# Seven products in the first MLP: two of three superblocks of a fused attention and MLP kernel

## The chip, the cores and the metric

The kernel runs on one core of a Trainium2 chip. The metric is device time in microseconds (us) of one execution; a smaller number is better.

## What is computed

Attention comes first: for 4 batches, 8 heads, 576 positions and 64 channels, the sum of a softmax attention over positions averaged in fours and of a local one with a band of 7 positions. Its output, as 2304 tokens of 512 channels, goes through two MLPs, all in float32:

```python
x = attn_out.transpose(0, 2, 1, 3).reshape(B * S, H * D)     # 2304 x 512
a = x @ w1;  b = x @ w2                                      # 512 -> 1024
y = ((a * b) @ w3) @ w_out                                   # 1024 -> 1024 -> 512
h = maximum(maximum(y @ u1, y @ u2), y @ u3)                 # 512 -> 768
out = h @ u_out                                              # 768 -> 512
```

## The kernel before, in words

Everything is kept transposed, channels on the 128 partitions and tokens along the free axis; `xy` holds the 2304 tokens of x, then of y, in four planes. Every float32 product is made of three TensorE matmuls on halves: an operand is split into a rounded high part (ScalarE, a copy into fp32r, L1033) and the rest (GpSimd, sometimes VectorE: a subtraction, L1187 or L784), and `split_product` (L596 to L598) adds high by high, high by low and low by high in PSUM. One operand is the stationary weight tile of 128 by 128, the other streams.

The work runs in three stages.

- **Prologue.** w3 @ w_out is formed once, as `w3o` (`product`), in 64 pieces of three matmuls, while the attention of the first batch (units 0 to 3, a unit is two heads of one batch) runs between the pieces.
- **First MLP**, five blocks of tokens, four of 512 and one of 256 (`T0`, `TN`). Of each block, L1 makes a and b (`first_mlp`, kind "L1": 8 tiles f of 128 hidden channels, twice for w1 and w2, 4 tiles k of the inner dimension, three matmuls each: 192), ScalarE copies a into `gate` (`gate_copy`), VectorE multiplies it by b (L856, `gate_product`), ScalarE and GpSimd split the product into `h_t`; L2 (96 matmuls) multiplies by `w3o` and ScalarE writes y over x. The attention units 4 to 15 are interleaved. A "part" is six matmuls of this stage.
- **Second MLP**, three superblocks of 768 tokens (`SUPER`, `HALF` = 384). Here each 2x2 block product of tiles is done with seven products instead of eight (`pair_products`): numbers e = 1 to 7, each of one summed weight tile and one summed operand. Products are added in PSUM and by VectorE. The summed and split weights are made once, in 24 steps n (`PREPS`), during the first MLP: SP loads 128 by 512 raw numbers (`load_raw`, L536), ScalarE copies them to PSUM (`copy_raw`), VectorE makes the four sums (L863 to L868, `combine`), ScalarE rounds (`high_wb`), VectorE subtracts (L784, `low_wb`), and SP stores 128 by 1792 numbers to DRAM in three DMAs (L545, `store_ready`). They are read back from there through a ring in `weights_split` (`load_group`, L558) in every superblock. The buffers of the steps lie in the memory of the attention, so `load_raw(0)` waits for the last unit (`x_ready`).

The order of the instructions on each engine is written out ahead of time: every job has a position, in parts of the stage, and each engine runs its own jobs sorted by position (`in_order`), waiting on semaphores. `position` gives it for the attention, `parts_of_mlp`, `after_parts` and `x_splits` for the MLP and `preparations` for the steps n. SP issues all DMAs, in its order too; a DMA whose wait isn't over holds up all DMAs behind it.

## Time and profile before

| | |
|---|---|
| median of 3 runs | 692.66 us (692.54 to 693.13) |
| the profiled execution | 692.93 us, span 691.1 us |
| TensorE busy | 684.6 us, 99% of the span |
| weight loads, beside the matmuls | 609.5 us |
| VectorE, ScalarE, GpSimd busy | 378.9, 244.0, 263.5 us |
| DMA | 131.73 MB, mean 191 GB/s |

The 1.8 us between the span and the device time lie ahead of the first and behind the last instruction. A matmul row's own duration holds its way through the array and overlaps the next one's; what a matmul costs TensorE is the distance between two starts.

### The profile page before, as it was taken

The numbers are of one execution on the slowest core, as the hardware profiler recorded it, in microseconds if no ns is written. First come the engines' busy times: TensorE is split into PE (matmuls) and PEld (weight loads), VectorE is DVE, ScalarE is ACT, GpSimd is POOL, SyncE is SP. The second block draws the span as 40 slices with busy tenths as digits, with TensorE's granted clock in tenths as the row PEclk, the third lists the DMA queues.
The fourth block names the chain that finished last, engine by engine and source line by source line (L and its number), as shares of the span: only waits on it lengthen the run. The fifth ranks groups of instructions, "written<-read, shape, count | busy, mean of one in ns | idle before, by whom it ended". The sixth has DMA issues, their size and how long they took to land.

```text
span 691.1 us, 15782 instructions
## 1 busy us (share of the span) xinstructions
PE 684.6 (99%) x6656; PEld 609.5 (88%) x6656; DVE 378.9 (55%) x707; ACT 244.0 (35%) x514; POOL 263.5 (38%) x240
## 2 busy tenths in 40 slices
PE   9999999999999999999999999999999999999998
PEld 7787788888888888888888999999999999999997
DVE  4464555433544354435666326676576767756673
ACT  5565333323333233245665334122431223412231
POOL 6989422410415112240222137123570335904341
PEclk9999999999999999999999999999999999999999
DMA  9884122222212222049999666777399765897732
GB/s 314 272 281 137 55 78 78 63 93 60 79 44 77 78 69 65 24 135 324 340 325 319 239 226 243 248 233 263 121 360 354 229 251 162 319 372 252 233 119 92
DMA packets 43798, 131.73 MB, mean 191 GB/s; under 512 B 4944, under 2 KB 8272, under 8 KB 42960
## 3 DMA queue, kind: packets, MB, share of 16 engines
q1 hardware_dynamic: 43728, 130.73, 55.4%
q8 instruction: 52, 0.85, 0.5%
q14 instruction: 18, 0.15, 0.1%
HBM read 103.97 MB, written 26.74 MB: 189 GB/s over the span
## 4 chain that ended last, share of the span: by engine, by line
PE 95%; POOL 3%; DMA 1%; DVE 0%; issue 0%; SPq 0%; ACT 0%; DVEq 0%
PE psum L596 29%; PE psum L597 28%; PE psum L598 28%; PE psum L635 3%; PE psum L613 2%; PE psum L606 2%; POOL second_split L1187 2%; PE psum L644 1%; PE psum L623 1%; DMA xy<-wa 1%; POOL product_split L1187 1%; POOL weights_split L1187 1%; DVE sums L939 0%; POOL attention L1191 0%; SPq L513 0%
## 5 line engine op out<-in xcount | busy, mean ns | idle before, releaser
L596 PE MATMUL psum<-second_split,weights_split 128*128 128x384 f32 x402 | 135.1, 336 | 2.3 <-issue 0.9
L598 PE MATMUL psum<-second_split,weights_split 128*128 128x384 f32 x402 | 134.3, 334 | 0.0
L597 PE MATMUL psum<-second_split,weights_split 128*128 128x384 f32 x402 | 134.3, 334 | 0.0
L1187 POOL TENSOR_TENSOR h_split<-gate,h_split 128x512 fp32r<-128x512 f32 (+1 forms) x40 | 47.1, 1178 | 223.6 <-ACT h_split L1033 223.6
L1187 POOL TENSOR_TENSOR second_split<-xy,second_split 128x384 fp32r<-128x384 f32 x75 | 82.0, 1118 | 129.1 <-ACT second_split L1033 129.1
L596 PE MATMUL psum<-x_split,weights_split 128*128 128x512 f32 (+1 forms) x320 | 120.8, 377 | 0.0
L597 PE MATMUL psum<-x_split,weights_split 128*128 128x512 f32 (+1 forms) x320 | 117.9, 369 | 0.0
L598 PE MATMUL psum<-x_split,weights_split 128*128 128x512 f32 (+1 forms) x320 | 117.9, 368 | 0.0
L596 PEld LDWEIGHTS psum<-second_split,weights_split 128*128 128x128 f32 x402 | 75.5, 188 | 4.5 <-issue 1.8
L597 PEld LDWEIGHTS psum<-second_split,weights_split 128*128 128x128 f32 x402 | 75.5, 188 | 0.0
L598 PEld LDWEIGHTS psum<-second_split,weights_split 128*128 128x128 f32 x402 | 75.5, 188 | 0.0
L596 PEld LDWEIGHTS psum<-x_split,weights_split 128*128 128x128 f32 x320 | 60.3, 189 | 11.8 <-issue 1.8
L598 PEld LDWEIGHTS psum<-x_split,weights_split 128*128 128x128 f32 x320 | 60.4, 189 | 10.3
L597 PEld LDWEIGHTS psum<-x_split,weights_split 128*128 128x128 f32 x320 | 60.4, 189 | 9.2
L856 DVE TENSOR_TENSOR gate<-gate,psum 128x512 f32<-128x512 f32 (+1 forms) x40 | 25.2, 631 | 69.4 <-PE psum L598 69.4
L1033 ACT ACTIVATE attention<-psum 128x896 fp32r<-128x896 f32 (+2 forms) x56 | 39.5, 706 | 61.7 <-PE psum L644 26.9
L596 PE MATMUL psum<-h_split,product_split 128*128 128x512 f32 (+1 forms) x160 | 59.8, 374 | 0.0
L597 PE MATMUL psum<-h_split,product_split 128*128 128x512 f32 (+1 forms) x160 | 58.9, 368 | 0.0
L598 PE MATMUL psum<-h_split,product_split 128*128 128x512 f32 (+1 forms) x160 | 58.9, 368 | 0.0
L1033 ACT ACTIVATE sums<-psum 128x384 f32<-128x384 f32 x33 | 16.2, 491 | 101.4 <-PE psum L598 101.3
L1033 ACT ACTIVATE second_split<-xy 128x384 fp32r<-128x384 f32 x75 | 37.7, 523 | 39.4 <-DVE xy L946 12.6
L1033 ACT ACTIVATE h_split<-gate 128x512 fp32r<-128x512 f32 (+1 forms) x40 | 23.5, 589 | 77.7 <-DVE gate L856 77.6
(111 smaller groups left out, 1157.1 us busy)
## 6 DMA issues: line engine op xcount, KB each, us to landing
weights_split<-weights_stream SPq DMA_DIRECT2D x39, 768.0 KB, 4.8
weights_split<-weights_stream SPq DMA_DIRECT2D x54, 512.0 KB, 4.8
weights_stream<-attention SPq DMA_DIRECT2D x48, 256.0 KB, 2.9
xy<-wa SPq DMA_DIRECT2D x40, 256.0 KB, 4.7
attention<-qk SPq DMA_DIRECT2D x16, 576.0 KB, 4.1
weights_stream<-attention SPq DMA_DIRECT2D x24, 384.0 KB, 3.2
weights_split<-weights_stream SPq DMA_DIRECT2D x6, 1152.0 KB, 5.1
attention<-v_win SPq DMA_DIRECT2D x16, 384.0 KB, 3.5
```

The lines of the kernel that those rows point to most:

```text
L596: pe.matmul(out, lhs[:, 0], rhs[:, 0], start=first, stop=False, skip_group_check=read_between)
L597: pe.matmul(out, lhs[:, 0], rhs[:, 1], start=False, stop=False, skip_group_check=read_between)
L598: return pe.matmul(out, lhs[:, 1], rhs[:, 0], start=False, stop=last, skip_group_check=read_between)
L606: mm = pe.matmul(score_d[rows, j, :], qkd[rows, 0, DSTEP * j:DSTEP * j + DROWS], qkd[rows, 1, :], start=True, stop=True)
L613: mm = pe.matmul(score_l[TW * i:TW * (i + 1), h, g, :], qk_sb[rows, 0, Q0[t]:Q0[t] + TW], qk_sb[rows, 1, K0[t]:K0[t] + TW], start=True, st ...
L623: mm = pe.transpose(turned_d[:, kt, P * j:P * (j + 1)], prob_d[:, j, TD * kt:TD * (kt + 1)], ident)
L635: mm = pe.matmul(bank(4 + i)[D * h:D * (h + 1), PV + TQ * g:PV + TQ * (g + 1)], v_sb[rows, g, D * h:D * (h + 1)], prob_t[rows, h, g, own:o ...
L644: mm = pe.matmul(pv_down[D * h:D * (h + 1), :], vd[:, kt, D * h:D * (h + 1)], own, start=kt == 0, stop=kt == 1)
L856: dve.tensor_tensor(at, at, bank(2 * (f % 2) + 1)[:, 0:TN[n]], ALU.mult).then_inc(h_ready, 1)
L1033: return act.activation(out, src, ACT.Copy)
L1187: return pool.tensor_tensor(out, full, high.bitcast(F32), ALU.subtract)
```

## The change

The first MLP's L1 uses seven products too, for tokens 768 to 2303 (superblocks 2 and 3). Tokens 0 to 767 stay plain, in two blocks of 384 (`SUPER`, `HALF`, `T0`, `TN`, `NB`). In these lines PROLOGUE is 64, PARTS 48, so `G_BEGIN` is 160 and `B_BEGIN` 336; for each of the two gated superblocks there are 56 parts of products (`GUNITS` = 8 units, 4 pairs of hidden tiles by w1 and w2, of 7 products of six matmuls), then 32 of L2.

```diff
-T0 = [0, 512, 1024, 1536, 2048]
-TN = [512, 512, 512, 512, 256]
-NB, TMAX = len(T0), 512
+SUPER, HALF = 3, 384
+T0 = [0, HALF]
+TN = [HALF, HALF]
+NB, TMAX = len(T0), HALF
...
+GP = F1 // 2
+GUNITS = 2 * GP
+GPREPS = GUNITS * KP
+GATED = SUPER - 1
+PRODUCT_W = 2 * KP * P
+PLACES = 9
+GMADE = 3
...
+G_ORDER = ((0, 1), (0, 2), (1, 4), (0, 6), (1, 3), (0, 5), (0, 7))
...
+G_BEGIN = PROLOGUE + PARTS * NB
+G_FIRST, G_PARTS = 7 * GUNITS, 7 * GUNITS + 8 * JO
+B_BEGIN = G_BEGIN + G_PARTS * GATED
...
-VISITS = {"S": 0, "T": 5, "V": 8}
+VISITS = {"S": 0, "T": 5, "V": 8.1}
+
+UNIT_AT = [None] * PAIRS + [PROLOGUE + 1.5 + 9.8 * i for i in range(2 * PAIRS)] + [
+    G_BEGIN - 5 + 15 * i for i in range(PAIRS)]
...
+def gate_preparations(late):
+
+    return [PROLOGUE + 5 + 4.9 * n + late for n in range(GPREPS)]
...
-    return [PROLOGUE + PARTS * 2 + 33.5 + 2.6 * n + late for n in range(PREPS)]
+    return [G_BEGIN + 54 + 3.35 * n + late for n in range(PREPS)]
...
+def gated_loads():
+
+    return [(G_BEGIN - 7 if i < PLACES else G_AT[PRODUCTS[i - PLACES]] + 1.15, ("PRODUCT", i)) for i in range(len(PRODUCTS))]
...
+            def load_gate_raw(n):
+                if n >= GMADE:
+                    sp.wait_ge(gmade_out[(n - GMADE) % 2], GMADE_INC * ((n - GMADE) // 2 + 1))
+                sp.dma_start(gmade_b[n % GMADE].rearrange("p (e two) c -> p e two c", two=2)[:, :, 1, :],
+                             wc[n].rearrange("p (e c) -> p e c", e=4)).then_inc(wc_in[n % GMADE], 16)
+
+            def store_gate(n):
+                to = products_dram(n // KP, n % KP)
+                sp.wait_ge(wc_hi, n + 1)
+                for r in range(2):
+                    some = slice(4 * r, min(4 * r + 4, 7))
+                    sp.dma_start(to[:, 0, some, :], ghigh_b[n % 2][:, r, 0:some.stop - some.start, :].bitcast(F32)).then_inc(
+                        gmade_out[n % 2], 16)
+                sp.wait_ge(wc_lo, n + 1)
+                sp.dma_start(to[:, 1], gmade_b[n % GMADE][:, 0:7, :]).then_inc(gmade_out[n % 2], 16)
+
+            def load_product(i):
...
+                if i >= PLACES:
+                    sp.wait_ge(product_done, i - PLACES + 1)
...
+                sp.dma_start(places[i % PLACES].bitcast(F32), product_dram(7 * (q % GUNITS) + IN_PIECE.index(e))).then_inc(
+                    place_in[i % PLACES], 16)
...
+            for step in in_order(loads(), gated_loads(),
+                                 [(max(at, PROLOGUE + 1), ("GATE_RAW", n)) for n, at in enumerate(gate_preparations(-4.5))],
+                                 [(at, ("GATE_OUT", n)) for n, at in enumerate(gate_preparations(5.5))],
+                                 [(at, ("RAW", n)) for n, at in enumerate(preparations(-4.5))],
+                                 [(at, ("READY", n)) for n, at in enumerate(preparations(4))]):
+                run[step[0]](*step[1:])
...
+            def gate_product(q, e):
...
+                pe.wait_ge(place_in[i % PLACES], 16 * (i // PLACES + 1))
...
+                for kp in range(KP):
+                    if u == 0:
+                        pe.wait_ge(xs_lo, 7 * KP * s + X_SPLIT[(e, kp)] + 1)
+                    mm = split_product(out, lhs[:, kp], xs_r[(e, kp)], kp == 0 and e in (1, 2, 5), kp == KP - 1, True)
+                mm.then_inc(product_done, 1)
...
+            def gate_result(q, tile):
...
+                if tile == (1, 0):
...
+                    dve.tensor_tensor(to, to, a, ALU.mult).then_inc(g_summed[tile], 1)
+                    return
...
+                if q % 2 == 0:
+                    wait_for_results(dve, q)
+                    dve.tensor_tensor(to, kept, from_bank, ALU.add).then_inc(g_summed[tile], 1)
+                else:
+                    dve.tensor_tensor(kept, kept, from_bank, ALU.add).then_inc(g_summed[tile], 1)
+                    dve.wait_ge(g_summed[tile], q + 1)
+                    dve.tensor_tensor(to, to, kept, ALU.mult).then_inc(gated_by[tile], 1)
...
+            def combine_wc(n):
+
+                made = gmade_b[n % GMADE]
+                pool.wait_ge(wc_in[n % GMADE], 16 * (n // GMADE + 1))
+                pool.tensor_tensor(made[:, 2, :], made[:, 7, :], made[:, 5, :], ALU.add)
...
+            def low_wc(n):
+                made = gmade_b[n % GMADE].rearrange("p (r e) c -> p r e c", r=2)
+                pool.wait_ge(wc_hi, n + 1)
+                low(made.bitcast(F32R), made, ghigh_b[n % 2]).then_inc(wc_lo, 1)
```

Beside what is shown: the sums of w1 and w2 for the seven products are made in 16 steps (`GPREPS`) during the two plain blocks. Each loads 128 by 512 numbers, GpSimd makes four sums and, after ScalarE has rounded (`high_wc`), the low parts; three DMAs store 128 by 1792 numbers to `gate_weights_stream` in DRAM. `load_product` reads 128 by 512 numbers for each of the 112 products into one of nine places, and product i + 9 can only be loaded when product i is done. Every product is loaded anew for superblock 3. The seven operands of x are made for each gated superblock (`split_xs`, `make_x`: 14 copies, 14 subtractions, 8 differences). ScalarE copies products 1, 6 and 7 (and every second 4) out of PSUM (`keep`), and VectorE adds and multiplies (`gate_result`). The gated h goes to `gated_r`, and L2 takes it in eight groups of 384 tokens (`last_layer`).

SP, in the products of superblock 3. L545 and L768 are `store_ready` before and now, L536 and L759 `load_raw`, L752 is `load_product`. Before:

```order
L545 DMA weights_stream<-attention 128x512 [waits wb_lo]
L545 DMA weights_stream<-attention 128x768
L545 DMA weights_stream<-attention 128x512
L536 DMA attention<-wb 128x512 [waits s_made]
L545 DMA weights_stream<-attention 128x512 [waits wb_lo]
```

and now:

```order
L768 DMA weights_stream<-attention 128x512
L752 DMA weights_split<-gate_weights_stream 128x512 [waits product_done]
L759 DMA attention<-wb 128x512 [waits s_made]
L752 DMA weights_split<-gate_weights_stream 128x512 [waits product_done] x2
L768 DMA weights_stream<-attention 128x512 [waits wb_lo]
L768 DMA weights_stream<-attention 128x768
L768 DMA weights_stream<-attention 128x512
L752 DMA weights_split<-gate_weights_stream 128x512 [waits product_done]
```

The loads of products now stand between the stores of the steps n. From the first load of superblock 3's second nine to the end of the steps there are 47 product loads, 14 steps' stores and 12 raw loads.

VectorE, in the same place. L1094 is `low_wb`, L1177 to L1182 are `combine`, L1238, L1248 and L1250 `gate_result`. Before (L784 is `low_wb`, L863 to L868 `combine`):

```order
L784 TENSOR_TENSOR attention<-psum,attention 128x7x128 [waits wb_hi]
L863 TENSOR_TENSOR psum<-psum,attention 128x128 [waits raw_copied]
L864 TENSOR_TENSOR psum<-psum,attention 128x128
L866 TENSOR_TENSOR psum<-psum,attention 128x128 [waits s1_made]
L868 TENSOR_TENSOR psum<-attention,psum 128x128 [waits s2_made]
```

and now:

```order
L1094 TENSOR_TENSOR attention<-psum,attention 128x7x128 [waits wb_hi]
L1238 TENSOR_TENSOR xy<-xy,psum 128x384 [waits g21_kept,product_done]
L1177 TENSOR_TENSOR psum<-psum,attention 128x128 [waits raw_copied]
L1178 TENSOR_TENSOR psum<-psum,attention 128x128
L1180 TENSOR_TENSOR psum<-psum,attention 128x128 [waits s1_made]
L1182 TENSOR_TENSOR psum<-attention,psum 128x128 [waits s2_made]
L1248 TENSOR_TENSOR gate<-gate,psum 128x384 [waits product_done,kept16]
L1250 TENSOR_TENSOR xy<-xy,gate 128x384 [waits g12_summed]
```

The results of the products, for which TensorE waits, now stand behind `low_wb`, which waits for ScalarE.

## Rows read from the trace of the kernel before

**Rows 1.** The page: busy time and, in 40 slices, the granted clock.

```profile
PE 684.6 (99%) x6656; PEld 609.5 (88%) x6656; DVE 378.9 (55%) x707; ACT 244.0 (35%) x514; POOL 263.5 (38%) x240
...
PEclk9999999999999999999999999999999999999999
```

**Rows 2.** Who TensorE waited for: total us, times, longest.

```profile
PE psum L720 <- DVE gate L900: 1.1, 1, 1.1
PE psum L596 <- issue: 0.9, 1, 0.9
PE psum L596 <- POOL second_split L1187: 0.8, 2, 0.4
PE psum L596 <- DVE sums L939: 0.6, 3, 0.2
```

**Rows 3.** Timeline, TensorE, 512 columns, from 295.76: start us, us.

```profile
295.76 0.39 PE L598 MATMUL psum<-x_split,weights_split 128*128 128x512 f32 x1
...
301.88 0.39 PE L598 MATMUL psum<-h_split,product_split 128*128 128x512 f32 x1
```

**Rows 4.** The same in the second MLP, 384 columns.

```profile
429.73 0.33 PE L596 MATMUL psum<-second_split,weights_split 128*128 128x384 f32 x1
...
433.89 0.33 PE L596 MATMUL psum<-second_split,weights_split 128*128 128x384 f32 x1
```

**Rows 5.** The same in the block of 256 tokens.

```profile
397.42 0.28 PE L598 MATMUL psum<-x_split,weights_split 128*128 128x256 f32 x1
...
408.58 0.28 PE L598 MATMUL psum<-x_split,weights_split 128*128 128x256 f32 x1
```

**Rows 6.** The chain that ended last: start us, us, what.

```profile
50.39 1.08 PE psum L635 x71
51.47 0.64 PE psum L644 x8
...
53.71 0.88 PE psum L606 x12
54.59 0.95 PE psum L613 x63
...
59.89 0.66 PE psum L623 x6
...
412.10 12.28 POOL second_split L1187 x10
```

**Rows 7.** Windows: us, busy of each engine, clock, DMA share, GB/s.

```profile
core 0: us, PE busy (x) PEld busy (x) DVE busy (x) ACT busy (x) POOL busy (x), PEclk, DMA share, GB/s
3.00:17.00 14.00, 13.90 (x167) 11.65 (x166) 7.52 (x15) 7.96 (x18) 10.31 (x9) 1.00 1.04 363
69.00:295.00 226.00, 225.98 (x3364) 182.30 (x3363) 104.39 (x205) 71.34 (x174) 65.40 (x58) 1.00 0.22 66
...
320.00:370.00 50.00, 50.00 (x222) 41.42 (x221) 33.17 (x78) 28.52 (x46) 10.67 (x9) 1.00 0.95 332
514.00:529.00 15.00, 14.11 (x81) 13.82 (x81) 7.01 (x14) 1.36 (x3) 1.96 (x3) 1.00 1.03 407
```

**Rows 8.** Groups by shape, VectorE: busy us, mean ns, idle before.

```profile
L946 DVE TENSOR_TENSOR xy<-xy,sums 128x384 f32<-128x384 f32 x54 | 36.2, 671 | 1.9
L784 DVE TENSOR_TENSOR attention<-psum,attention 128x896 fp32r<-128x896 f32 x24 | 26.2, 1092 | 26.3 <-ACT attention L1033 26.3
...
L976 DVE TENSOR_TENSOR sums<-sums,psum 128x384 f32<-128x384 f32 x18 | 9.9, 552 | 7.9 <-PE psum L598 7.9
...
L868 DVE TENSOR_TENSOR psum<-attention,psum 128x128 f32<-128x128 f32 x24 | 7.1, 296 | 0.8
```

**Rows 9.** The same, GpSimd.

```profile
L1187 POOL TENSOR_TENSOR h_split<-gate,h_split 128x512 fp32r<-128x512 f32 x32 | 41.2, 1288 | 192.4 <-ACT h_split L1033 192.4
...
L1187 POOL TENSOR_TENSOR h_split<-gate,h_split 128x256 fp32r<-128x256 f32 x8 | 5.9, 737 | 31.3 <-ACT h_split L1033 31.3
```

**Rows 10.** Who SP's DMA queue waited for: total us, times, longest.

```profile
SPq L545 <- DVE attention L784: 36.2, 24, 2.3
```

372 lines of the change are left out of this document (337 added, 35 removed), and 2 rows, old and new, of the table FOLLOWS.

## The prediction

> **What bounds the kernel now.** I read the page first: TensorE is busy 99% of the span and its granted clock stands at full speed in every slice [rows 1]. Then who TensorE waited for: 0.9 us, 0.8 us in two waits, 0.6 us in three, and the start [rows 2]. So no transfer and no other engine sets the time. It is the sum of TensorE's matmuls, and a change is worth what it takes from that sum, less the waits that it makes.
>
> What a matmul costs is read from starts in the timeline. 512 columns: (301.88 - 295.76) / 27 = 0.2267 us [rows 3]. 384 columns: (433.89 - 429.73) / 24 = 0.1733 us [rows 4]. 256 columns: (408.58 - 397.42) / 93 = 0.1200 us [rows 5]. The three lie on one line: 0.4167 ns a column and 13.3 ns for each matmul. Narrower matmuls thus cost something by themselves.
>
> **TensorE's sum.** Removed are the five blocks of the first MLP: 4 x 288 matmuls of 0.2267 us and 288 of 0.12 us, 261.1 + 34.6 = 295.7 us. In their place stand two plain blocks, 2 x 288 x 0.1733 = 99.8 us, and two gated superblocks of 336 + 192 matmuls, 2 x 528 x 0.1733 = 183.0 us, in all 282.9 us. The difference is **-12.8 us**. (The product saves 36,864 columns, 15.4 us; 192 more matmuls give 2.6 us back.) Attention, prologue and second MLP keep their matmuls.
>
> The wait of 0.8 us on GpSimd's splits ahead of the second MLP [rows 2, 6] should go: there a chain of ten splits, 12.28 us, followed the last block's h. Now y of superblock 1 is ready from the plain blocks, and most of the 14 splits have positions beside the L2 of superblock 3, 32 parts of 1.04 us. **-0.6 us** on the path; between 0 and -0.8.
>
> **The DMA in superblock 3** is the term that decides. A product uses its weights for one part, 6 x 0.1733 = 1.04 us, and loads 128 x 512 numbers, 0.262 MB. Alone that is 252 GB/s. In superblock 2 the loads of the attention come on top; units stand 15 parts apart, in time 15 x 1.04 + 4.2 = 19.8 us with their own five groups of matmuls (1.08, 0.64, 0.88, 0.95 and 0.66 us, [rows 6]), and move 1.31 MB each (128 x 1152, 128 x 768 and 80 x 1024 numbers): 66 GB/s more. 320 GB/s should pass.
>
> The 24 steps that make the second MLP's weights (0.262 MB read, 0.917 MB stored each) start only after the attention. Before, they ran beside plain blocks: [rows 7] show 332 GB/s and 0.95 of the DMA engines at 320 to 370 us, that is one step per 3.55 us. Now the first ten fall beside the L2 of superblock 2, where TensorE loads nothing, and the other fourteen between the products of superblock 3. SP's order ties them together: a product's load stands behind the stores whose position is earlier.
>
> Follow superblock 3 from position 89, where its first product is done and the tenth can be loaded, to position 141, where product 53 starts: 52 parts, 54.1 us of TensorE. Ahead of product 53 the queue must have moved 45 product loads (11.8 MB), the stores of 13 steps (11.9 MB) and 12 raw loads (3.1 MB): **26.9 MB**, 497 GB/s. No window of the trace has that. What it has: 363 GB/s with rows of about 2 KB a partition and a full queue at 3 to 17 us, 407 GB/s with ring groups of 4 to 6 KB at 514 to 529 us, both with a share of over 1.0 [rows 7]. The steps' window gives 332 / 0.95 = 349 GB/s at full share, and the loads at the start 363 / 1.04 = 349 as well. The new product loads have 2 KB a partition, the stores 2 and 3 KB, so the start's window is nearest, and I take 363 GB/s: 26.9 / 0.363 = 74.1 us, a wait of **+20.0 us**. Bounds: 407 GB/s gives 66.1 us and +12.0; 332 GB/s, the steps' own rate, gives 81.0 us and +26.9. Nine places hold 9.4 us of work, but they are full at position 88 and so are within these numbers; the products go back to one per 1.04 us only when the steps are out.
>
> This term rests on two rates that TensorE never met before, since the ring groups are long and read far ahead. The Trainium skill ("HBM Reference", Specifications (TRN2)) says that a core streaming alone gets about 425 GB/s. The trace has 407 over 15 us for loads alone and less for every stretch with stores; by the page's figure the wait would be an estimated 9 us and the whole about 690.5 us.
>
> **What else the change adds.** VectorE, in the same 52 parts: 13 steps of 1.09 + 4 x 0.296 = 2.27 us, 29.6 us; and for each 14 parts (a pair of units) seven operations on PSUM at 0.55 us and three in SBUF at 0.67 us, 5.9 us, so 21.8 us [rows 8]. 51.4 us of 54.1: it would just fit, and under 74 us of DMA it is covered. If the DMA cover were gone, VectorE would be at 95% and late wherever it waits for ScalarE; that is a part of the rest term below.
>
> GpSimd, in the plain blocks: 256 columns take 0.737 us and 512 take 1.288 [rows 9], so 2.15 ns a column and 0.19 us. A step of the w1, w2 sums has four operations of 128 columns (0.46 us each) and one of 1024 (2.39): 4.2 us. With h, x and the attention's sums about 6.5 us in a step's 4.9 parts, which last 5.1 us and 2.1 us of attention. 0.9 of its time, mostly off the path: h's last tile stands ahead of the next long operation in its order.
>
> The DMA there: 16 steps of 1.18 MB and 8 units of 1.31 MB, 29.4 MB in 78.4 parts and 8 units, 115 us: 256 GB/s. But the stores write pieces of 512 bytes, which no row shows. From below: no wait at 332 GB/s. From above: attention alone shows 66 / 0.22 = 300 GB/s at full share [rows 7], 98 us, still no wait. From the two saturated windows I estimate some 20 ns a row beside the bytes, hence 215 GB/s for such stores and 110 us in all. It stays inside, narrowly.
>
> The attention's chain: in the prologue the turned scores follow 4.35 us behind the scores (55.54 to 59.89) with no wait [rows 2, 6]. Now five parts, 5.2 us, lie between. In two places only one part lies between a unit's values and the next scores; some 0.5 us each.
>
> For these together, **+2 us**, between 0 and 6.
>
> **Sum.** 692.9 (the profiled execution) - 12.8 - 0.6 + 20.0 + 2.0 = 701.5 us. The profiled execution lies 0.3 us over the median of the runs, so I say 701 us: slower. 0.2%, 1.4 us, is about what a measurement of this kernel can tell from no change.
>
> **The rivals.**
> 1. *The queue runs at its ring rate.* Then the wait is 9 to 12 us and the others are small: 692.9 - 13.4 + 12 + 1 = 692.5, down to 690 by the page's rate. For: 407 GB/s was held for 15 us. Against: those were reads of long rows. 17%.
> 2. *Stores and loads hardly hinder each other*, and the sign turns: reads are 14.9 MB and writes 11.9 MB; if only the greater counted, 14.9 / 0.363 = 41 us, under TensorE's 54.1. No wait there, 692.9 - 13.4 + 2 = 681.5. It decides once stores and loads together pass 497 GB/s. For: no window has both directions saturated. Against: the steps' window has 0.95 of the engines busy at 332 GB/s, three quarters of it stores. 12%.
> 3. *The queue is also left empty.* SP waits for `low_wb` before a step's stores, 36.2 us in 24 steps, 1.5 us each [rows 10], and the product loads behind are held up with it; `low_wb` on VectorE and the `gate_result` behind it wait for ScalarE, which waits for older stores. If the queue runs dry half that time, 14 x 0.75 = 10.5 us more: 712; all of it: 722. The small stores of the first steps, if slower than estimated, would end there too. 16%.
> 4. The forecast, 696 to 709: 55%.
>
> **Range and chances.** Rival 2 (12%) and the upper half of rival 3 (8%) are left out: 690 to 714 us. Faster by over 0.2%: rival 2 and a third of rival 1, 18%. Within 0.2%: 8%. Slower: 74%.
>
> **What would show it.** Right: TensorE waits summing to some 20 us between 88 and 146 parts of the stage, released by DMA into `weights_split` from `gate_weights_stream`, in short waits ahead of products, while the DMA share is near 1.0 and the rate 350 to 410 GB/s; TensorE's matmul counts as above and none longer; hardly a wait in superblock 2. Wrong: TensorE waits small there with a rate near 500 GB/s (rival 2); waits released by VectorE or ScalarE with a DMA share under 0.9 (rival 3); a granted clock under 1.0 where TensorE waits, which would make each product longer by an amount that no row here prices.

## The result, and the profile after

The changed kernel takes **719.46 us** (median of 4 runs, 716.67 to 720.53), the kernel before on the same chip 692.89 us (692.54 to 693.20). The ratio is 1.0377, 95% interval 1.0347 to 1.0407: slower, by 26.6 us, where 701 us was forecast. The profiled execution took 716.67 us, its span is 714.9 us (691.1 before).

The page of the changed kernel. Where TensorE was busy for 99% it is now for 96%, its granted clock is no longer full everywhere [rows 1], and the queue moves 180 MB in place of 132:

```profile
PE 686.9 (96%) x6848; PEld 654.2 (92%) x6848; DVE 416.4 (58%) x779; ACT 275.2 (38%) x590; POOL 342.8 (48%) x344
...
PEclk9999999999999999998998899999999999999999
...
GB/s 309 270 280 127 139 248 258 195 247 210 207 242 208 257 262 219 274 299 315 371 406 408 347 217 195 183 258 229 229 227 404 245 221 228 243 404 251 211 144 88
```

Windows over the three parts of the program (columns as in [rows 7]). The first product of superblock 3 starts at 328.79, the second MLP at 447.50. The fourth window begins with the stretch for which the prediction worked out its bytes and ends at 408.0, where the queue runs empty; product 53, the end of that stretch, starts at 411.1:

```profile
0.00:328.79 328.79, 319.75 (x4808) 292.77 (x4809) 188.24 (x369) 156.88 (x355) 215.96 (x223) 0.99 0.77 238
328.79:447.50 118.71, 103.35 (x529) 99.65 (x529) 57.29 (x123) 50.30 (x95) 30.53 (x30) 0.91 0.85 321
447.50:714.90 267.40, 263.75 (x1513) 261.76 (x1512) 170.85 (x289) 68.05 (x140) 96.28 (x91) 1.00 0.68 238
329.80:408.00 78.20, 62.84 (x299) 59.14 (x298) 46.62 (x105) 38.23 (x69) 12.12 (x12) 0.88 1.03 386
```

What each part should take is known. Before, the second MLP began at 424.42; less the 12.8 us of the prediction's first term it should begin at 411.6, and superblock 3, 528 matmuls of 0.1733 us, 91.5 us, should begin at 320.1. So the 23.8 us that the span grew, and the 12.8 us that were saved and lost again, 36.6 us, lie here:

| part | should take | takes | more | TensorE idle |
|---|---|---|---|---|
| up to superblock 3 | 320.1 | 328.8 | 8.7 | 9.0 |
| superblock 3 | 91.5 | 118.7 | 27.2 | 15.4 |
| second MLP | 266.7 | 267.4 | 0.7 | 3.7 |

Idle is the window less TensorE's busy time; in the first and last row a part of it stood there before as well (6.5 us in all). In superblock 3 it leaves 11.8 us that TensorE spent in slower matmuls. Of the 9.0 us idle in the first row, 8.1 lie ahead of 220 us, in the prologue and the plain blocks; the first product of superblock 2 starts at 218.87.

Who TensorE waited for, in place of [rows 2]:

```profile
PE psum L861 <- ACT attention L1392: 6.4, 4, 3.0
PE psum L822 <- issue: 4.8, 3, 4.0
PE psum L822 <- DVE results L1238: 3.0, 1, 3.0
PE psum L822 <- DVE xy L1238: 2.6, 1, 2.6
PE psum L822 <- ACT gate L1392: 2.3, 2, 2.0
PE psum L822 <- ACT parts L1392: 1.8, 4, 0.9
```

No row names a DMA. In superblock 3 TensorE waits for `gate_result` (L1238) and for ScalarE's copies of products (`parts`, `gate`), that is for the banks of PSUM into which the next products go. The first row is the attention's values (L861), in the plain blocks.

The longest wait, 3.98 us, is one of the three under `issue`, for which the profile names no releaser. TensorE's timeline there, at the first wait of superblock 3 (start, us, what, in brackets the idle time ahead):

```profile
330.53 0.33 PE L823 MATMUL psum<-weights_split 128*128 128x384 f32 x1
330.70 0.34 PE L824 MATMUL psum<-weights_split 128*128 128x384 f32 x1
335.02 0.66 PE L822 MATMUL psum<-weights_split 128*128 128x384 f32 x1 [3.98 <-issue]
335.48 0.52 PE L823 MATMUL psum<-weights_split 128*128 128x384 f32 x1
335.80 0.52 PE L824 MATMUL psum<-weights_split 128*128 128x384 f32 x1
```

Two losses stand here. One is the wait. ScalarE's timeline shows what it was for: `high_wb`, waiting for an older store, stood ahead of the copy of a product into `parts`, which ended at 334.91, 0.1 us ahead of TensorE's start:

```profile
333.62 0.92 ACT L1392 ACTIVATE attention<-psum 128x896 fp32r<-128x896 f32 x1 [2.04 <-DMA weights_stream<-attention]
334.43 0.48 ACT L1392 ACTIVATE parts<-psum 128x384 f32<-128x384 f32 x1
```

The other is in the starts behind the wait: 0.32 us apart, where 0.17 us is the full rate. The granted clock of 330 to 340 us was 0.70, a mixture of the full clock and the lower level of 1.2 GHz. Such starts stand in five stretches: behind the waits that ended at 335.02, 358.21 and 378.39 (3.98, 3.05 and 2.59 us), and from 391.85 and 405.31 on, behind shorter waits (1.97 us until 390.73, 1.58 and 0.24 until 405.31). Together they took 9.0 us more than at the full rate. Four windows of 10 us:

```profile
330.00:340.00 10.00, 6.02 (x22) 5.73 (x22) 5.53 (x12) 4.67 (x8) 0.00 (x0) 0.70 0.96 318
350.00:360.00 10.00, 5.77 (x27) 4.90 (x26) 6.88 (x16) 5.08 (x9) 2.03 (x2) 0.89 1.04 394
...
370.00:380.00 10.00, 7.04 (x35) 6.35 (x34) 6.66 (x16) 5.04 (x9) 1.84 (x2) 0.91 1.05 407
390.00:400.00 10.00, 9.24 (x43) 8.98 (x44) 7.46 (x19) 5.87 (x11) 2.48 (x3) 0.83 1.05 404
```

The busy time of TensorE hides this loss, since a slow matmul is busy too: it is in the 118.7 - 91.5 - 15.4 = 11.8 us. These windows also show the DMA engines fully busy at 404 to 407 GB/s with reads and stores mixed.

The chain that ended last, 348 to 379 us (start, us, what). It goes round in the steps that make the second MLP's weights: the stores land, ScalarE rounds the step after next (`high_wb`), VectorE subtracts (`low_wb`, L1094), SP stores (L768). `ready_b` has two buffers, so one round carries two steps:

```profile
348.42 7.06 DMA weights_stream<-attention
355.56 0.93 ACT attention L1392
356.51 1.10 DVE attention L1094
...
358.67 6.73 DMA weights_stream<-attention
...
368.55 7.11 DMA weights_stream<-attention
...
378.64 7.31 DMA weights_stream<-attention
```

A round takes (378.64 - 348.42) / 3 = 10.1 us. The order plans two steps in 2 x 3.35 parts of 1.04 us, 7.0 us. If all seven rounds for the fourteen steps that lie here took as long as these three, they come to 7 x 3.1 = 21.7 us, an estimate: most of the 27.2. The products' copies and sums stand in the same orders as the steps, so TensorE is slowed to the steps' pace.

In the plain blocks another chain ends last. GpSimd works without a gap, ScalarE waits for it with the rounding of the w1, w2 sums, and the unit's `attention` copy, for which TensorE waits 2.96 us, stands behind:

```profile
188.19 2.35 POOL room L1615
190.54 0.97 POOL weights_split L1615
...
192.96 0.46 POOL room L1659
...
193.44 0.03 ACT xy L1392
...
194.91 0.70 ACT attention L1392
...
195.75 1.14 PE psum L861 x69
```

ScalarE's own waits say the same for the whole run:

```profile
ACT attention L1392 <- DMA weights_stream<-attention: 26.9, 14, 3.1
ACT xy L1392 <- POOL room L1659: 26.7, 12, 5.1
```

### The profile page after: what moved, and what is told of

Read it like the earlier page. It is cut to its first block, busy times and chain, and to the rows that moved or that the text cites. A ratio compares the mean times of both kernels' runs of the same rounds, so it can differ in the third digit from the quotient of the medians.

```text
span 714.9 us, 16905 instructions
## 1 busy us (share of the span) xinstructions
PE 686.9 (96%) x6848; PEld 654.2 (92%) x6848; DVE 416.4 (58%) x779; ACT 275.2 (38%) x590; POOL 342.8 (48%) x344
## 4 chain that ended last, share of the span: by engine, by line
PE 82%; DMA 6%; POOL 4%; DVE 2%; issue 2%; ACT 2%; SPq 1%; ACTq 0%; DVEq 0%; POOLq 0%
PE psum L822 25%; PE psum L824 24%; PE psum L823 24%; DMA weights_stream<-attention 5%; PE psum L861 2%; PE psum L839 2%; PE psum L832 2%; PE psum L870 1%; POOL room L1615 1%; PE psum L849 1%; ACT attention L1392 1%; DMA attention<-ident 1%; POOL h_split L1615 1%; DVE attention L1094 1%; SPq L768 1%
## 5 line engine op out<-in xcount | busy, mean ns | idle before, releaser
L1615 POOL TENSOR_TENSOR second_split<-xy,second_split 128x384 fp32r<-128x384 f32 x99 | 103.1, 1058 | 224.8 <-ACT second_split L1392 224.8
L822 PE MATMUL psum<-weights_split 128*128 128x384 f32 x278 | 99.1, 357 | 16.2 <-issue 4.8
L823 PE MATMUL psum<-weights_split 128*128 128x384 f32 x278 | 96.8, 348 | 0.0
L824 PE MATMUL psum<-weights_split 128*128 128x384 f32 x278 | 96.5, 347 | 0.0
L1615 POOL TENSOR_TENSOR weights_split<-xy,weights_split 128x384 fp32r<-128x384 f32 (+1 forms) x65 | 76.3, 1190 | 21.4 <-ACT weights_split L1392 21.3
L822 PEld LDWEIGHTS psum<-weights_split 128*128 128x128 f32 x278 | 55.2, 198 | 21.8 <-issue 21.4
L1392 ACT ACTIVATE second_split<-xy 128x384 fp32r<-128x384 f32 x99 | 49.4, 521 | 41.5 <-DVE xy L1305 12.6
L823 PEld LDWEIGHTS psum<-weights_split 128*128 128x128 f32 x278 | 55.0, 198 | 0.0
L824 PEld LDWEIGHTS psum<-weights_split 128*128 128x128 f32 x278 | 55.0, 198 | 0.0
L822 PE MATMUL psum<-x_split,weights_split 128*128 128x384 f32 x128 | 45.4, 354 | 0.0
L1094 DVE TENSOR_TENSOR attention<-psum,attention 128x896 fp32r<-128x896 f32 x24 | 26.2, 1090 | 30.2 <-ACT attention L1392 30.2
L824 PE MATMUL psum<-x_split,weights_split 128*128 128x384 f32 x128 | 43.3, 339 | 0.0
L823 PE MATMUL psum<-x_split,weights_split 128*128 128x384 f32 x128 | 43.3, 338 | 0.0
L1392 ACT ACTIVATE xy<-psum 128x384 f32<-128x384 f32 x45 | 22.0, 489 | 55.1 <-PE psum L824 51.2
```

What stands on the lines that cost most here:

```text
L822: pe.matmul(out, lhs[:, 0], rhs[:, 0], start=first, stop=False, skip_group_check=read_between)
L823: pe.matmul(out, lhs[:, 0], rhs[:, 1], start=False, stop=False, skip_group_check=read_between)
L824: return pe.matmul(out, lhs[:, 1], rhs[:, 0], start=False, stop=last, skip_group_check=read_between)
L1094: return dve.tensor_tensor(out, full, high.bitcast(F32), ALU.subtract)
L1392: return act.activation(out, src, ACT.Copy)
L1615: return pool.tensor_tensor(out, full, high.bitcast(F32), ALU.subtract)
```

## The experiments

Each kernel is the changed one with the edit shown. Beside the median I give the length of superblock 3 (from its first product to the second MLP) in the profiled execution, since it is freer of what happens elsewhere: where the plain blocks are the same, superblock 3 began at 328.8, 329.7, 332.2, 330.3, 333.7, 332.9 and 332.5 us, a scatter of 5 us that the medians contain. TensorE was idle for 8.8 to 10.3 us up to there in all seven, so the rest of the scatter is in slower matmuls. The profiled execution of the change is the fastest of its four. The kernel before took 692.5 to 693.0 us each time.

| kernel | median us (runs, range) | ratio, 95% interval | superblock 3: us | of it idle | slower matmuls |
|---|---|---|---|---|---|
| the change | 719.46 (4, 716.67 to 720.53) | 1.0377 (1.0347 to 1.0407) | 118.7 | 15.4 | 11.8 |
| quarter of each product load | 709.42 (4, 707.87 to 713.17) | 1.0250 (1.0211 to 1.0288) | 110.4 | 11.5 | 7.3 |
| sums on VectorE | 730.03 (4, 729.19 to 736.34) | 1.0557 (1.0511 to 1.0603) | 119.7 | 15.5 | 12.7 |
| later rounding | 721.40 (4, 718.30 to 724.57) | 1.0413 (1.0373 to 1.0453) | 121.4 | 21.5 | 8.5 |
| steps spread | 701.86 (4, 700.88 to 708.79) | 1.0152 (1.0102 to 1.0202) | 97.6 | 3.2 | 2.9 |
| product loads of 16 partitions | 707.42 (4, 707.05 to 710.03) | 1.0219 (1.0195 to 1.0242) | 107.0 | 9.8 | 5.7 |
| half of the low parts on GpSimd | 712.16 (4, 711.14 to 714.11) | 1.0282 (1.0259 to 1.0305) | 119.0 | 15.0 | 12.5 |
| spread, slower w1, w2 sums | 699.35 (4, 696.01 to 703.30) | 1.0110 (1.0056 to 1.0163) | 97.9 | 3.7 | 2.7 |
| and earlier steps | 698.81 (4, 697.90 to 699.41) | 1.0085 (1.0068 to 1.0102) | 98.0 | 3.6 | 2.8 |
| tuned, first | 695.38 (10, 693.05 to 698.68) | 1.0042 (1.0022 to 1.0062) | 99.4 | 5.9 | 1.9 |
| tuned, second | 694.83 (11, 692.85 to 696.23) | 1.0019 (1.0006 to 1.0032) | 100.8 | 6.6 | 2.7 |
| no steps beside products | 724.38 (3, 723.37 to 728.94) | 1.0467 (1.0430 to 1.0503) | 92.9, then a wait of 23.9 | 1.0 | 0.4 |
| step stores of 16 partitions | 702.75 (4, 700.65 to 705.56) | 1.0147 (1.0108 to 1.0186) | 99.7 | 6.0 | 2.2 |

The last column is the length less 91.5 us less the idle time. Some 2 to 3 us of it stand there even where the granted clock was 1.00 throughout (small stores, tuned), so the clock's own part in the change is nearer 9 than 12 us.

**1. Fewer bytes in the product loads.** First, in superblock 3 only a quarter of the columns:

```diff
-                sp.dma_start(places[i % PLACES].bitcast(F32), product_dram(7 * (q % GUNITS) + IN_PIECE.index(e))).then_inc(
-                    place_in[i % PLACES], 16)
+                w = PRODUCT_W if i < GUNITS * 7 else PRODUCT_W // 4
+                sp.dma_start(places[i % PLACES][:, 0:w].bitcast(F32),
+                             product_dram(7 * (q % GUNITS) + IN_PIECE.index(e))[:, 0:w]).then_inc(place_in[i % PLACES], 16)
```

> Of each product load of superblock 3 only the first quarter of the columns is moved (the other three quarters of a place keep older numbers, so tokens 1536 to 2303 are computed with wrong weights). Orders, counts and waits of all engines stay; 9.2 MB leave the DMA queue between the first product and the end of the steps. Theory A (bytes: the queue holds too many of them there): 26.9 MB become 18.1, 44 us at 407 GB/s under 54 us of TensorE; the 15.4 us of TensorE waits in 328.8 to 420 us of the changed kernel fall under 4, its clock there stays near 1.00, so the 11.8 us of slow matmuls go too: the time falls by 20 to 27 us, to 692 to 699 us. Theory B (the order: rounding of the steps stands ahead of the copies that TensorE waits for): the waits stay above 10 us, the time falls by less than 8 us.

It took 709.42 us, and superblock 3 110.4 us: 8.3 us less. The DMA engines were still busy for 0.88 to 0.91 of each 20 us between 320 and 400, at about 300 GB/s. That is neither a free queue nor a full one, and settles little, so the same was done with whole rows in fewer partitions:

```diff
+                rows = P if i < GUNITS * 7 else 16
+                sp.dma_start(places[i % PLACES][0:rows, :].bitcast(F32),
+                             product_dram(7 * (q % GUNITS) + IN_PIECE.index(e))[0:rows, :]).then_inc(place_in[i % PLACES], 16)
```

> Of each product load of superblock 3 only 16 of the 128 partitions are moved, in full rows of 2 KB (the rest of a place keeps older weights, so tokens 1536 to 2303 are computed with wrong weights). The quarter loads still held the DMA share at 0.9 with rows of 512 bytes; this takes 10.8 MB and their time out of the queue. Orders and waits of all engines stay. Theory A (the full queue alone): the share falls under 0.75 beside the products, TensorE's waits there fall from 15.4 us to under 3, and the time to 690 to 697 us. Theory B (beside the queue's load, ScalarE's and VectorE's copies and sums for TensorE stand behind high_wb and low_wb, which wait for older stores or for the copy of raw numbers even in a queue that isn't full): waits of 6 to 11 us stay and the time is 702 to 710 us.

707.42 us, superblock 3 107.0 us. The chain that ended last, two of its stores between 370 and 396 us:

```profile
370.51 3.24 DMA weights_stream<-attention
...
392.52 3.32 DMA weights_stream<-attention
```

These stores land in 3.2 and 3.3 us instead of 7 (the one ahead of them took 4.8; the median of the 256 KB stores between 328 and 408 us is 2.9), and 11.7 us are gone. The other 15.5 us of the 27.2 stay although the product loads hardly weigh: 9.8 us of idle time and the median are inside theory B's bands. The DMA share between 320 and 400 us was still 0.86 at 297 GB/s, not under 0.75 as theory A had it.

**2. The steps' stores made small.** The twin of the last one: the loads whole, the stores of 14 steps cut to 16 partitions (and their reading in the second MLP).

```diff
+                    rows = P if n < 10 else 16
-                    sp.dma_start(group_dram(GROUP_OF[(u, es[0])])[:, words * kp:words * (kp + 1)],
-                                 ready_f[n % 2][:, at:at + words]).then_inc(made_out[n % 2], 16)
+                    sp.dma_start(group_dram(GROUP_OF[(u, es[0])])[0:rows, words * kp:words * (kp + 1)],
+                                 ready_f[n % 2][0:rows, at:at + words]).then_inc(made_out[n % 2], 16)
...
```

> The fourteen steps beside superblock 3 (n of 10 and more) store only 16 of their 128 partitions, 0.115 MB in place of 0.917 MB, and the second MLP reads only those 16 partitions of these groups; the output there is not the reference's. The product loads, raw loads and all work on the engines stay. In the changed kernel superblock 3 takes 118.7 us where its matmuls alone take 91.5, and two steps take 10.1 us there where the order plans 7.0. Theory A, the loop: what holds TensorE is that a step waits until the stores of the step two before have landed, about 7 us in the full queue. With small stores the landing falls to some 3 us or less, two steps take 6.5 to 7 us, superblock 3 takes 92 to 98 us and the kernel 696 to 701 us. Theory B, the order of VectorE and ScalarE itself (a product's sum stands behind a step's low part, whatever a store takes), as the kernel with few rows of the products left 107 us: superblock 3 takes 105 to 109 us and the kernel 706 to 710 us. Theory C, mere bytes: as with few rows of the products, some 11 MB fewer, also about 107 us and a store landing of 3 us; B and C are told apart by the DMA share, under 0.7 in B with waits left, and over 0.85 in C.

702.75 us, superblock 3 99.7 us. The windows (columns as above), from 330 us:

```profile
330.00:340.00 10.00, 6.66 (x39) 6.37 (x38) 6.53 (x17) 5.92 (x10) 0.00 (x0) 1.00 0.98 324
...
360.00:370.00 10.00, 10.00 (x59) 9.71 (x57) 8.29 (x18) 6.31 (x11) 2.03 (x2) 1.00 0.95 321
```

19.0 us of the 27.2 are gone, more than with small loads, although both take away about 11 MB here (11.2 and 10.8); of the 8.2 us that stay, 3.3 are one wait at 338 us, where steps with whole stores still land. This is nearest to theory A, the loop of the steps, 1.7 us above its bands for superblock 3 and for the kernel. B's and C's 105 us and more didn't come, though the DMA share between 330 and 400 us, 0.86, is the one that C named. Of its lead over the small loads, 7.3 us, 3.5 are slower matmuls (2.2 against 5.7 us) and 3.9 idle time. What the two show together: bytes beside the products matter whichever they are, those of the steps more than those of the products. That the way of a store through the full queue is the link is what the chain shows; these two kernels don't separate it from the bytes, since the landing fell to about 3 us in both (medians of 2.9 us, and 3.5 for the small stores), and that of the whole product loads here to 4.5 us from 6.6.

**3. No steps beside the products.**

```diff
-    return [G_BEGIN + 54 + 3.35 * n + late for n in range(PREPS)]
+    at = [54 + 3.35 * n for n in range(10)] + [146 + 3.35 * n for n in range(14)]
+    return [G_BEGIN + a + late for a in at]
-    return [((at - 4 if i < 2 else at + 5.5 + 1.1 * i) + late, step) for i, step in enumerate(Y_STEPS)]
+    return [(at + 52 + 0.8 * i + late, step) for i, step in enumerate(Y_STEPS)]
```

> The changed kernel with no step beside the products of superblock 3: ten beside the L2 of superblock 2 and fourteen behind the products, reaching past the first MLP's end; the splits of y come behind them. Whatever the cause, bytes or order, it needs the steps there: TensorE's waits and the lower clock between the first and the last product of superblock 3 must vanish (under 1 us, clock 1.00, DMA near 252 GB/s). If they don't, the products hold themselves up (copies of ScalarE, sums of VectorE, the nine places), and neither theory is right. The time is paid at the end: fourteen steps of 3.3 to 3.5 us against 32 us of L2, and 14 splits with 8 differences behind them, 15 us: 20 to 35 us of waits ahead of the second MLP, 708 to 722 us in all.

The kernel is slower, 724.38 us, 2 us over the expected range, but superblock 3 itself takes 92.9 us of the 91.5 that its matmuls need. One of its windows, and what TensorE waited longest for:

```profile
360.00:380.00 20.00, 20.00 (x117) 20.00 (x117) 7.93 (x14) 6.83 (x14) 5.07 (x5) 1.00 0.80 255
```

```profile
PE psum L823 <- DMA weights_split<-weights_stream: 23.9, 1, 23.9
```

So the products with their own loads hold up nobody; 25.8 of the 27.2 us come from the steps beside them. And the steps can't simply go elsewhere: put behind the products they aren't ready when the second MLP begins (a wait of 6.2 us for GpSimd's splits of y follows the 23.9). Their chain there, without any product in it, shows what a round is worth alone:

```profile
423.45 4.20 DMA weights_stream<-attention
...
443.60 2.86 DMA weights_stream<-attention
```

Two more such stores lie between these, so (443.60 - 423.45) / 3 = 6.7 us for two steps, just inside the 7.0 that the change's order plans. The three landings took 3.7 us on average here and 7.0 in the change: the plan has no room for the 3.2 us between them.

**4. Rounding later.** Could the order be mended by letting the step's jobs stand further back, so that the store has landed when ScalarE comes to them?

```diff
-                                 [(at, ("HIGH_WB", n)) for n, at in enumerate(preparations(1.6))],
+                                 [(at, ("HIGH_WB", n)) for n, at in enumerate(preparations(3.6))],
-                                 [(at, ("LOW_WB", n)) for n, at in enumerate(preparations(2.1))],
+                                 [(at, ("LOW_WB", n)) for n, at in enumerate(preparations(4.1))],
-                                 [(at, ("READY", n)) for n, at in enumerate(preparations(4))]):
+                                 [(at, ("READY", n)) for n, at in enumerate(preparations(5.5))]):
```

> high_wb and low_wb of the steps come two parts later in the orders of ScalarE and VectorE, the stores one and a half parts later; bytes and counts stay. Theory A (bytes): the queue is as full as before, the time changes by less than 3 us. Theory B (order): ScalarE and VectorE stand less behind the landing of older stores, TensorE waits in superblock 3 fall by more than 6 us and the time by 8 to 20 us.

No gain: 721.40 us, superblock 3 121.4 us, and TensorE waits for ScalarE's `parts` 9.3 us in seven waits where it was 1.8 in four. That is theory A's outcome, a change of less than 3 us. I read it so that a loop that is too slow isn't made faster by entering it later.

**5. The steps spread.** Ten at the old pace in superblock 2's L2, eight at 6.9 parts beside the products, six in superblock 3's L2:

```diff
-    return [G_BEGIN + 54 + 3.35 * n + late for n in range(PREPS)]
+    at = [54 + 3.35 * n for n in range(10)] + [90 + 6.9 * n for n in range(8)] + [141 + 3.1 * n for n in range(6)]
+    return [G_BEGIN + a + late for a in at]
-    return [((at - 4 if i < 2 else at + 5.5 + 1.1 * i) + late, step) for i, step in enumerate(Y_STEPS)]
+    return [(at + 16.5 + 0.75 * i + late, step) for i, step in enumerate(Y_STEPS)]
```

> The steps keep their start, but run at 3.35 parts only beside the L2 of superblock 2 (ten), at 6.9 parts beside the products of superblock 3 (eight) and at 3.1 parts beside its L2 (six); the splits of y for the second MLP come later for it. Theory A: beside the products the queue now needs 252 GB/s and 1.18 MB per 7.2 us, 416 GB/s, close to the 407 measured: TensorE's waits there fall from 15.4 to 1 to 5 us with the clock mostly up; 20 us are gained, of which up to 6 are given back ahead of the second MLP, where 14 splits of 1.1 us on GpSimd now begin only some 15 parts before it: 698 to 706 us. Theory B: the waits fall only with the number of steps there, from 15.4 to about 9, and the time is 705 to 715 us.

701.86 us. The window of superblock 3:

```profile
330.31:427.89 97.58, 94.39 (x530) 91.07 (x530) 59.68 (x122) 48.25 (x90) 25.28 (x24) 1.00 0.95 351
```

97.6 us instead of 118.7: the same steps, the same bytes for each, only eight of them beside the products instead of fourteen. 17.6 us of the 26.6 are back by positions alone. The queue wasn't empty for it:

```profile
350.00:400.00 50.00, 49.13 (x275) 47.00 (x274) 31.62 (x69) 26.86 (x50) 12.18 (x12) 1.00 0.99 369
```

In these 50 us TensorE was idle for 0.9 us, 0.2 of it for a product load; in the change it was idle for 9.6 us there, at a share of 1.05 and 404 GB/s. The product loads took as long to land (medians 6.7 and 6.8 us), the steps' 256 KB stores 5.1 us instead of 6.2. So a busy queue with slow landings doesn't by itself hold TensorE: two steps have 2 x 6.9 parts here, 14.4 us, and their round fits.

**6. The sums of w1 and w2.** For the plain blocks the question was whether GpSimd's load holds the attention. The sums were moved to VectorE (`combine_wc` as in the change, with `dve` in place of `pool`):

```diff
-                pool.tensor_tensor(made[:, 2, :], made[:, 7, :], made[:, 5, :], ALU.add)
+                dve.tensor_tensor(made[:, 2, :], made[:, 7, :], made[:, 5, :], ALU.add)
```

> The four sums of each of the 16 steps for w1 and w2 are made by VectorE and no longer by GpSimd; nothing else. Theory C (GpSimd, busy 0.8 to 0.97 of the time in the plain blocks, holds up ScalarE's high_wc and behind it the copies that the attention's values wait for): TensorE's waits for ScalarE ahead of the values, 6.4 us in 4, fall under 1.5 us, and the slow matmuls behind them go: the time falls by 6 to 9 us. Rival (the step's stores of 512-byte pieces or the attention's own chain set it): the waits stay above 4 us and the time falls by less than 3 us.

Slower still, 730.03 us; superblock 3 starts 11.9 us later than in the change and takes 119.7 us, 1.0 more. VectorE's groups by shape (busy us, mean ns) show why:

```profile
L1257 DVE TENSOR_TENSOR room<-room 128x128 f32<-128x128 f32 x16 | 20.3, 1266 | 0.0
L1256 DVE TENSOR_TENSOR room<-room 128x128 f32<-128x128 f32 x16 | 13.3, 833 | 0.0
...
L1261 DVE TENSOR_TENSOR room<-room 128x128 f32<-128x128 f32 x16 | 7.8, 489 | 0.5
```

Sums of the same shape with an operand in PSUM took 296 ns [rows 8], and the same four took 0.46 us each on GpSimd. Why they were so slow can be read in the same trace, from the two engines' timelines between 60 and 230 us. The 24 of the 64 sums beside which GpSimd ran nothing took 0.28 to 0.29 us each; the other 40 took 1.10 us on average and up to 2.47. Two of them:

```profile
85.10 2.47 DVE L1257 TENSOR_TENSOR room<-room 128x128 f32<-128x128 f32 x1
117.77 0.28 DVE L1257 TENSOR_TENSOR room<-room 128x128 f32<-128x128 f32 x1
```

During the first GpSimd made the low parts, 84.99 to 87.42 us, and it was idle during the second. The move says little of GpSimd's load: GpSimd's busy time between 60 and 215 us fell from 125.2 to 86.9 us, but VectorE became late, and TensorE's wait ahead of the values rose from 6.4 to 9.2 us. So a part of GpSimd's work was left out instead, half of the subtraction that makes the low parts:

```diff
-                low(made.bitcast(F32R), made, ghigh_b[n % 2]).then_inc(wc_lo, 1)
+                low(made[:, 0].bitcast(F32R), made[:, 0], ghigh_b[n % 2][:, 0]).then_inc(wc_lo, 1)
```

> low_wc makes the low parts of four of the eight 128-column pieces only (products 1, 4, 7 and the fourth piece of the order get no low weights, so tokens 768 to 2303 are inexact): GpSimd has 1.1 us less in each of the 16 steps of w1 and w2 and nothing else changes. Theory C (GpSimd is what holds ScalarE and the attention in the plain blocks; the run with the sums on VectorE failed because VectorE's operations in SBUF took 0.5 to 1.3 us there): TensorE's 6.4 us of waits ahead of the values fall under 3 us, and the time falls by 3 to 8 us against the changed kernel, to 711 to 716 us. Rival (the order of ScalarE alone): no change within 2 us.

712.16 us. Superblock 3 starts at 322.7 us, 6.1 us earlier, and takes 119.0 us, as in the change. The values' wait, 6.4 us in the change:

```profile
PE psum L861 <- ACT attention L1392: 2.5, 3, 1.2
```

GpSimd's busy time between 60 and 215 us fell from 125.2 to 112.4 us of 155. The start lies 6.1 us below the lowest of the seven starts above, more than they scatter, and TensorE's idle time up to there is 5.3 us, where the seven had 8.8 to 10.3. So GpSimd is what costs most of the 8.7 us up to superblock 3.

**7. Towards a version that wins.** Spread steps, and the w1, w2 sums at another pace:

```diff
-    return [PROLOGUE + 5 + 4.9 * n + late for n in range(GPREPS)]
+    return [PROLOGUE + 4 + 5.4 * n + late for n in range(GPREPS)]
```

> The spread steps of the run before (e4_spread), and the 16 steps of w1 and w2 5.4 instead of 4.9 parts apart, begun one part earlier. Theory C: GpSimd's load per step falls from 0.9 to 0.85 of the time and ScalarE waits less; TensorE's waits ahead of the values fall from 6.4 to 2 to 5 us, and the time to 697 to 701 us from 701.9. Rival (the positions of single steps against the attention's decide, not the load): waits move but their sum stays within 1.5 us.

699.35 us, with runs from 696.0 to 703.3. Next, the last attention units closer together (11.6 parts in place of 15) and two steps drawn ahead to 44 parts:

```diff
-    G_BEGIN - 5 + 15 * i for i in range(PAIRS)]
+    G_BEGIN - 5 + 11.6 * i for i in range(PAIRS)]
...
+    at = [44 + 5.3 * n for n in range(2)] + [54.6 + 3.35 * n for n in range(10)] + [91 + 7.3 * n for n in range(7)] + [141 + 3.1 * n for n in range(5)]
...
+    return [(at + 14 + 0.8 * i + late, step) for i, step in enumerate(Y_STEPS)]
```

> As the slower sums, and the last four attention units 11.6 parts apart instead of 15, so that the steps of the second MLP's weights can begin ten parts earlier: two stand beside the products of superblock 2, ten beside its L2, seven beside the products of superblock 3, five beside its L2. Theory A: with 0.9 times the steps' rate beside the products of superblock 3 the waits there fall by 1 to 2 us, and the splits of y get two parts more: 694 to 700 us. Rival: the denser attention units make VectorE, with sums and products of superblock 2, late: waits of 3 us and more between 220 and 290 us, 700 to 706 us.

698.81 us: no clear gain over the one ahead. Then two versions from the waits that were left:

```diff
-    G_BEGIN - 5 + 15 * i for i in range(PAIRS)]
+    G_BEGIN - 5 + 13.3 * i for i in range(PAIRS)]
...
+    at = [4 + 5 * n for n in range(6)] + [37.5 + 5.3 * n for n in range(10)]
+    return [PROLOGUE + a + late for a in at]
...
+    at = [49.5 + 3.6 * n for n in range(11)] + [91 + 6.6 * n for n in range(8)] + [141 + 3 * n for n in range(5)]
+    return [G_BEGIN + a + late for a in at]
...
+    return [(at + 13.9 + 0.8 * i + late, step) for i, step in enumerate(Y_STEPS)]
```

> Orders alone are changed, in three places: the 16 steps of w1 and w2 leave out the stretch where block 1's x is split and stand so that h's last tile comes ahead of them on GpSimd; the last four attention units stand 13.3 parts apart and the steps of the second MLP's weights begin 4.5 parts earlier, eleven of them ahead of superblock 3's products, eight beside them, five beside its L2; the splits of y start 2.6 parts earlier than in the spread version. If the three waits seen in the slower-sums run (2.7 us for x_out at 134, 2.8 us for h at 201, 2.5 us ahead of the second MLP at 427) are mishaps of position, they go: 688 to 693 us, level with or below the kernel before. If they only move: 695 to 701 us.

695.38 us in 10 runs (693.05 to 698.68), inside the band for waits that only moved. And with the units at 15 again and the steps of the fifth experiment slightly closer:

```diff
+    at = [54 + 3.35 * n for n in range(10)] + [90 + 6.5 * n for n in range(8)] + [139.5 + 3 * n for n in range(6)]
...
+    return [(at + 14.9 + 0.8 * i + late, step) for i, step in enumerate(Y_STEPS)]
```

> As the tuned version, but with the attention units 15 parts apart as in the changed kernel, ten steps ahead of superblock 3's products, eight beside them at 6.5 parts and six behind. If the start of superblock 3 suffers from a denser attention (as in the early-steps run, 3.2 and 2.8 us there), this one is the faster by 2 to 4 us: 687 to 692 us. If the end (splits of y, 1.33 us each of the differences on VectorE beside GpSimd) decides, it is the slower by 1 to 3 us.

694.83 us in 11 runs, 24.6 us less than the change. The two orders that were weighed against each other can't be told apart by 695.38 and 694.83 us. At a ratio of 1.0019 (1.0006 to 1.0032) this one is still 0.2% above the kernel before; none of the versions beat it. Its windows up to superblock 3 and over it:

```profile
0.00:326.06 326.06, 319.20 (x4808) 292.46 (x4809) 188.36 (x369) 157.05 (x355) 216.46 (x223) 0.99 0.77 240
326.06:426.86 100.80, 94.25 (x529) 91.03 (x529) 61.39 (x122) 50.05 (x94) 28.60 (x26) 1.00 0.97 353
```

6.0 us stay ahead of superblock 3 and 9.3 in it, 15.3 us against the 12.8 that the products save.

## Why the prediction was right or wrong

**TensorE's sum, -12.8: it fits.** The matmuls stand 0.1733 us apart wherever the clock is full, and with the steps out of the way superblock 3 took 92.9 of 91.5 us.

**-0.6 ahead of the second MLP: plausible, not separable.** No wait for GpSimd's splits stands there in the list of the change; the second MLP itself took 0.7 us more, which I haven't explained.

**The step that failed: TensorE's wait in superblock 3 taken as bytes over rate, +20.0.** It came out at +27.2, and by the prediction's own stretch as well: from 329.8 us to product 53 at 411.1, 81.3 us, where 54.1 was TensorE's sum and 74.1 the forecast. Its place holds: the steps beside the products cost nearly all of it (third experiment), and the DMA engines' share was 1.03. But TensorE didn't wait for the bytes of the product loads. It waited, through ScalarE and VectorE, for the steps' loop, 10.1 us for two steps where 7.0 were planned, and it lost some 9 us of the 27.2 to the lower clock.

Both factors of the sum were off too, and in opposite directions. The queue held 404 GB/s for the 50 us from 350 on, so "the start's window is nearest", 363, chose the wrong row. The bytes were 30.2 MB until 408.0, not 26.9: the list of this stretch has the stores of the last fifteen steps (46 DMAs; the count had 13 steps), 47 product loads (45) and 13 raw loads (12).

```profile
weights_split<-gate_weights_stream SPq DMA_DIRECT2D x47, 256.0 KB, 6.6
weights_stream<-attention SPq DMA_DIRECT2D x31, 256.0 KB, 5.6
weights_stream<-attention SPq DMA_DIRECT2D x15, 384.0 KB, 5.8
attention<-wb SPq DMA_DIRECT2D x13, 256.0 KB, 6.6
```

With the bytes measured and 404 GB/s the formula gives 30.2 / 0.404 - 54.1 = 20.7 us, nearly the +20.0 again: that the two errors cancel is luck, and the other 6.5 us aren't in it. (With the stretch's mean rate, 386 GB/s, it gives 24.1 us, but 30.2 / 0.386 is only the length of the window itself and explains nothing.) The clock was named at the end of the prediction and left without a price. Whether its 9 us would have been idle time otherwise, in a queue as full, isn't shown.

**How the wait reaches TensorE: not as said.** Waits for DMA into `weights_split`, released to the products, were to be seen; there is not one. The queue's fullness came back through the loop of landing, `high_wb`, `low_wb` and store, and TensorE waited for ScalarE and VectorE. That is the third rival's mechanism, but not its condition: that rival wanted a queue that runs empty, and its share was 1.03. It matters, since "the loads come too late" would call for more places, while what helped was fewer steps beside the products.

**Everything else, +2: too small.** It came out at +8.7. These 6.7 us, the 7.2 of the term above and 1.3 from the second MLP and the term of -0.6 make the 15.2 us between 701.5 and the profiled 716.67. GpSimd's 0.9 "mostly off the path" was the error: its share between 60 and 215 us was 0.81, but ScalarE's `high_wc` waits for it (26.7 us in 12 waits), and the attention's copies stand behind that. An order is as late as its latest job; a share tells how much an engine works, not who stands behind it. VectorE's 51.4 us were somewhat too many: it was busy 47.2 us between 329.8 and 411.1. The 512-byte stores can't be judged: the share was 0.64 between 60 and 120 us and 0.74 between 120 and 220, and no wait of TensorE names them.

**The rivals.** The ring's rate (1), 407 GB/s, was nearly reached, and the time still didn't follow: there were more bytes than counted, and TensorE waited for the loop. Of the Trainium skill's figure ("HBM Reference", Specifications (TRN2), about 425 GB/s for a core alone) the trace says that 404 to 407 were held for 50 us with stores mixed in, 4 to 5% under it. That stores and loads don't hinder each other (2) is refuted: 497 GB/s never occurred, and cutting either kind by some 11 MB gave 12 and 19 us.

**What stays open.** A third `ready_b` would let the loop turn at the same landing with half as much again in flight; it wasn't tried. How much of the 27.2 us is the loop's landing and how much mere bytes isn't settled either: both went down together wherever one was cut, and in the spread steps, where the queue stayed busy, the steps per microsecond fell with the rate. The scatter of 5 us in where superblock 3 begins, and the 0.7 us of the second MLP, are unexplained.

## What to carry to other kernels

Price a chain of load, compute and store by its round: landing plus engines plus issue, divided by its buffers, with the landing taken from a stretch in which the queue is as full as it will be. Here a plan of 7.0 us stood on a round of 6.7 us that became 10.1 us in a full queue. And when you fill an engine that others wait for in order, ask what stands behind each of its waits, not what share it is busy.

## What the runs showed of the hardware that I had not expected

- **Landing time grows with the queue's fill.** The same 0.26 MB store took 3.1 us before between 320 and 370 us, at a share of 0.95 [rows 7], and 6.2 us in the change between 350 and 400, at 1.05 and 404 GB/s (medians of 28 and 20). A fifth more throughput came with twice the latency.
- **A wait costs more than itself.** After waits of 3.98, 3.05 and 2.59 us in superblock 3, and 1.1 us after one of 1.97 and behind one of 1.58 too, TensorE's granted clock was at 1.2 GHz for some microseconds (matmuls 0.32 us apart), and the stretch lost some 9 us so, beside 15.4 us of idle time. It wasn't so every time: behind a wait of 3.34 us in the kernel with small stores the clock stayed full, which is a part of that kernel's lead. The Trainium skill ("TensorE: Matmul & The Clock Gate", What's actually happening) has the two levels as a gate that follows how busy TensorE has been; that the lower level stands behind waits agrees with it.
- **VectorE pays for operands in SBUF while GpSimd works.** With both inputs in SBUF, 128 by 128 sums took 0.28 to 0.29 us where GpSimd ran nothing beside them and 1.10 us on average, up to 2.47, where it did (sixth experiment); with one input in PSUM they took 0.296 us on average [rows 8]. The Trainium skill ("SBUF — State Buffer", SBUF: two separate sides) says that VectorE with two SBUF inputs and a GpSimd operation that reads SBUF lock each other out for a whole instruction. The rows agree: the sum of 2.47 us ended just after GpSimd's operation of 2.43 us.
